# The moving operand of the 512-column matmuls read in runs of 16 bytes out of order, in a convolution and two-layer MLP kernel on one core

## The reference

```
w = softmax(weight_gen)                       # per token and head, 7 taps
x = sum over k of w[k] * x_pad[token + k]     # 8192 x 192
h = maximum(x @ w_in, 0);  x = (h * h) @ w_out
h = x @ w_in2;  out = (h * clip(h + 3, 0, 6) / 6) @ w_out2
```

## Time and profile before

| | |
|---|---|
| time, median of 2 runs | 1127.13 us (1126.98 to 1127.29) |
| span of the profiled execution | 1125.2 us |
| TensorE (PE) busy, matmuls | 1119.4 us, 99%, 9940 records |
| weight loads (PEld) busy | 1082.5 us, 96% |
| VectorE (DVE) busy | 906.8 us, 81% |
| ScalarE (ACT) busy | 668.8 us, 59% |
| granted TensorE clock | 1.000 of full speed |
| DMA | 41.28 MB, mean 37 GB/s |

### The profile page before, as it was taken

One profiled execution on the slowest core, in us unless ns is written; L12 is line 12 of the kernel. 1 busy time (PEld: TensorE's weight loads), 2 busy tenths in 40 slices (PEclk: granted clock), 3 DMA queues, 4 the chain that ended last, 5 costly groups with the idle time before them and its releaser, 6 DMA issues.

```text
span 1125.2 us, 25509 instructions
## 1 busy us (share of the span) xinstructions
PE 1119.4 (99%) x9940; PEld 1082.5 (96%) x9940; DVE 906.8 (81%) x985; ACT 668.8 (59%) x747; POOL 3.1 (0%) x10
## 2 busy tenths in 40 slices
PE   9999999999999999999999999999999999999998
PEld 8998999999999999999999999999999999999997
DVE  8788796987969789697887978879698797976665
ACT  7986556565565655645556555555655556456554
POOL 1000000000000000000000000000000000000000
PEclk9999999999999999999999999999999999999999
DMA  7221002020110201103020020200202002010001
GB/s 214 86 66 36 6 16 63 4 74 7 30 48 3 75 6 57 25 0 77 4 66 15 0 77 4 70 11 8 69 4 73 8 17 59 0 40 4 1 16 29
DMA packets 79302, 41.28 MB, mean 37 GB/s; under 512 B 56172, under 2 KB 72300, under 8 KB 79272
## 3 DMA queue, kind: packets, MB, share of 16 engines
q1 hardware_dynamic: 79144, 40.64, 13.9%
q10 hardware_dynamic: 128, 0.22, 0.1%
HBM read 29.42 MB, written 11.40 MB: 36 GB/s over the span
## 4 chain that ended last, share of the span: by engine, by line
PE 99%; DVE 0%; DMA 0%; ACT 0%; issue 0%; DVEq 0%
PE h_ps L1131 46%; PE y_ps L1141 31%; PE y_ps L1149 21%; PE h_ps L988 0%; DMA wraw<-in_weight_gen_dram 0%; PE y_ps L1099 0%; PE y_ps L988 0%; PE y_ps L1272 0%; PE h_ps L1099 0%; PE y_ps L1253 0%; DVE prod L721 0%; PE y_ps L1254 0%; PE y_ps L1259 0%; PE y_ps L1256 0%; PE h_ps L1089 0%
## 5 line engine op out<-in xcount | busy, mean ns | idle before, releaser
L1131 PE MATMUL h_ps<-xt,win 64*128 64x512 f32 x4552 | 1026.4, 386 | 0.0
L1131 PEld LDWEIGHTS h_ps<-xt,win 64*128 64x128 f32 x4552 | 801.3, 184 | 14.9
L1141 PE MATMUL y_ps<-hid_hi,wout 64*128 64x512 f32 x2032 | 542.5, 386 | 0.0
L503 ACT ACTIVATE hid_hi<-hid 128x1024 fp32r<-128x1024 f32 x240 | 254.7, 1061 | 328.9 <-DVE hid L822 166.0
L831 DVE TENSOR_TENSOR hid_lo<-hid,hid_hi 128x1024 fp32r<-128x1024 f32 x253 | 309.5, 1223 | 147.6 <-ACT hid_hi L503 141.5
L1141 PEld LDWEIGHTS y_ps<-hid_hi,wout 64*128 64x128 f32 x2032 | 373.3, 184 | 7.1 <-PE y_ps L1141 0.3
L1141 PE MATMUL y_ps<-hid_lo,wout 64*128 64x512 f32 x1016 | 311.6, 386 | 0.0
L1149 PE MATMUL y_ps<-hid_hi,wout 64*128 64x512 f32 x1016 | 311.4, 386 | 0.0
L1149 PE MATMUL y_ps<-hid_lo,wout 64*128 64x512 f32 x1016 | 311.3, 386 | 0.0
L1141 PEld LDWEIGHTS y_ps<-hid_lo,wout 64*128 64x128 f32 x1016 | 186.8, 184 | 4.0 <-DVE hid_lo L806 0.3
L1149 PEld LDWEIGHTS y_ps<-hid_hi,wout 64*128 64x128 f32 x1016 | 186.9, 184 | 3.7 <-PE y_ps L1149 0.3
(11 more groups left out here) (116 smaller groups left out, 358.1 us busy)
## 6 DMA issues: line engine op xcount, KB each, us to landing
xwin<-in_x_dram SPq DMA_DIRECT2D x14, 960.0 KB, 5.9
by_feature<-stage SPq DMA_DIRECT2D x52, 96.0 KB, 2.0
out_dram<-outs SPq DMA_DIRECT2D x240, 16.0 KB, 1.5
out_dram<-outs SPq DMA_DIRECT2D x240, 8.0 KB, 1.4
stage<-by_feature SPq DMA_DIRECT2D x13, 256.0 KB, 3.0
stage<-in_moe_w_out_dram SPq DMA_DIRECT2D x8, 384.0 KB, 3.6
stage<-in_moe_w_in_dram SPq DMA_DIRECT2D x8, 256.0 KB, 3.7
stage<-in_moe_w_in_dram SPq DMA_DIRECT2D x16, 128.0 KB, 3.7
```

What stands on the lines that cost most here:

```text
L503: act.activation(hi, hid[:, slot], ACT.Copy).then_inc(hi_done, 1)
L1131: return pe.matmul(h_ps[:, s % 2, t, :], win[layer][r, wn, cols], src[r, xn, :], start=bool(rows) and n in (0, SHORT), stop=not rows and n ...
L1141: return pe.matmul(ps[:, 0, :], wout[layer][r, tile, w_cols], src, start=bool(rows) and s == 0 and n == 0, stop=not rows and s == STEPS - ...
```

## The change

Each moving operand of 512 columns is given with a different order of its values. Two helpers are added; a run is `LINE = 4` values of fp32, 16 bytes:

```diff
+    LINE = 4
+        def woven(tokens):
+            return tokens.rearrange("p (a b c) -> p b a c", a=2, c=LINE)
+        def unwoven(tokens):
+            return tokens.rearrange("p (b a c) -> p a b c", a=2, c=LINE)
```

```diff
-                return pe.matmul(sums_of(s, 0)[:, t, :], win[0][r, w, cols], xt[1][r, x, :], start=start, stop=stop,
+                return pe.matmul(sums_of(s, 0)[:, t, :], win[0][r, w, cols], woven(xt[1][r, x, :]), start=start, stop=stop,
...
-                return pe.matmul(h_ps[:, s % 2, t, :], win[layer][r, wn, cols], src[r, xn, :],
+                return pe.matmul(h_ps[:, s % 2, t, :], win[layer][r, wn, cols], woven(src[r, xn, :]),
...
-                return pe.matmul(ps[:, 0, :], wout[layer][r, tile, w_cols], src,
+                return pe.matmul(ps[:, 0, :], wout[layer][r, tile, w_cols], unwoven(src),
...
-                return pe.matmul(ps[:, 1, :], wout[layer][r, PAIR * s + t, HI_LO_REST], src,
+                return pe.matmul(ps[:, 1, :], wout[layer][r, PAIR * s + t, HI_LO_REST], unwoven(src),
...
-                                     xt[0][REST:P, 3, :], start=False, stop=stop, tile_position=(REST, 0))
+                                     woven(xt[0][REST:P, 3, :]), start=False, stop=stop, tile_position=(REST, 0))
```

More of the change, by code:

```diff
@@ L1252, in output_sums @@
                 for t, tile in enumerate(tiles):
-                    pe.matmul(main, w[:, tile, HI_MAIN], his[:, t, :], start=False, stop=False)
-                    pe.matmul(main, w[:, tile, LO_MAIN], his[:, t, :], start=False, stop=False)
+                    pe.matmul(main, w[:, tile, HI_MAIN], unwoven(his[:, t, :]), start=False, stop=False)
+                    pe.matmul(main, w[:, tile, LO_MAIN], unwoven(his[:, t, :]), start=False, stop=False)
                 for t, tile in enumerate(tiles):
-                    pe.matmul(rest, w[:, tile, HI_LO_REST], his[:, t, :], start=False, stop=False)
+                    pe.matmul(rest, w[:, tile, HI_LO_REST], unwoven(his[:, t, :]), start=False, stop=False)
                 pe.wait_ge(lo_done, g + 1)
                 for t, tile in enumerate(tiles):
-                    ins = pe.matmul(rest, w[:, tile, HI_LO_REST], los[:, t, :], start=False, stop=last and t == PAIR - 1)
+                    ins = pe.matmul(rest, w[:, tile, HI_LO_REST], unwoven(los[:, t, :]), start=False, stop=last and t == PAIR - 1)
                 if last:
@@ L1262, in output_sums @@
                 for t, tile in enumerate(tiles):
-                    ins = pe.matmul(main, w[:, tile, HI_MAIN], los[:, t, :], start=False, stop=last and t == PAIR - 1)
+                    ins = pe.matmul(main, w[:, tile, HI_MAIN], unwoven(los[:, t, :]), start=False, stop=last and t == PAIR - 1)
                 ins.then_inc(mm2_done, 1)
```

## The result

The changed kernel takes 1197.91 us (1197.56 and 1198.27) against 1127.13 us: a ratio of 1.063 with a 95% interval of 1.061 to 1.065, 70.8 us slower. The forecast was 1127 us in a range from 1095 to 1155 us. The direction was that of rival B, which had 0.16.

What follows compares the result with a forecast made beforehand. TensorE's 9708 matmuls of 512 columns, by their distance, were taken to bound the kernel. The only term, 4864 slots by the change of distance d, was put at 0, leaving 1127 us, range 1095 to 1155 us.

Steps and rivals of the forecast that it cites:

- rival B: TensorE's moving reads pause at each jump of address: 1386 us at one column each, 1250 or 1263 if one order pays; chance 0.16.
- It removes and adds no instruction ... So the sum has a single term: Whole kernel: 9708 matmuls before and after, so time is 1127.1 + 4.864 x d us, d the change of distance per slot in ns.
- a pair of row tiles takes 200 / 884 = 226.2 ns: TensorE's distance from 1768 matmuls in a 200 us window; 512 columns take 213.3 ns, an excess of 12.9 ns a pair.
- I take d = 0: TensorE's 512-column matmuls: the new read order was taken to leave the distance per slot unchanged, giving 1127 us.
- a pause is at least one column: Upper bound for TensorE's moving reads: 0.417 ns at each of 128 changes of run, +53.3 ns a slot, +259 us.
- The first row for d = 0: TensorE's transposes: 15 ns above their weight load, about the long matmuls' 12.9 ns, so the excess is per instruction, not reading.
- The second row: VectorE reads 224 values in one run or in 32 runs of 28 bytes, both in 392 ns: broken runs show no price.
- The rule of the Trainium skill: SBUF reads: 16-byte lines, full rate from two hits, a penalty per line change; 128 changes as before, so no added time.
- Rival C: Another read order serves TensorE better, giving back part or all of the excess: down to 1064 us; chance 0.12.
- Rival D: A small fixed price per matmul instruction for more pattern dimensions: 0 to +15 us, up to 1142 us; chance 0.08.
- if TensorE prepares its reads only along neighbouring lines: Sign that the forecast of no effect is wrong: TensorE readies the next read only where it lies in the neighbouring line.
- B would be fewer ... with L1131 beside L1149 telling which of the two orders pays: Sign of pauses at jumps: 1431 matmuls in 200 us, not 1768, at one column per run; the two lines' distances compared.

Runs made afterwards that it cites:

- line64: The changed kernel with runs of 64 values, 256 bytes, in place of runs of 4: 1127.11 us, ratio 1.000 against the kernel before the change.
- run 516: No run number: a TensorE-alone probe segment reading runs of 4 values in twos, the second 516 values behind the first; 227 ns a pair, as plain order.

## Why the prediction was wrong

- **What bounds the kernel**: right. The number of matmuls by their distance makes the time in all eight full kernels that were run, up to the waits just named; no step of the sum other than d was needed.
- **"It removes and adds no instruction ... So the sum has a single term"**, 4.864 x d: right. With d = 14.7 ns it gives 71.5 us; 70.8 us were measured.
- **"a pair of row tiles takes 200 / 884 = 226.2 ns"**: a slip in reading, without weight. The count holds matmuls in flight at the edge; the distance was 226.7 ns and the excess over the columns 13.4 ns, not 12.9.
- **"I take d = 0"**: the step that failed: the term was put at nothing. d is +23 ns for the woven reads and +5 for the unwoven where an order stands alone, and +14.7 ns a slot in the kernel.
- **The bound above, "a pause is at least one column" per change of run, +53.3 ns**: the bound held, but I treated it as the next price above nothing. 23 ns over 128 changes is 0.18 ns each, 5 ns is 0.04: less than a column slot each on average. The average says nothing of which changes pay. The text of rival B allowed "part of one", and named 0.036 ns per run as the point from which it decides; its priced values, 1250 to 1386 us, did not follow from that and left the space from 1155 to 1250 us to no case.
- **The first row for d = 0, an excess that doesn't grow with the columns "is a cost per instruction"**: that it doesn't grow is so from 256 to 512 columns (13 ns at 256, 384 and 512), though the transposes, whose 68 ns a pair no fp32r matmul of 64 columns reached (112 ns), could not show it. The conclusion that order can't change it is refuted in both directions: 2.5 ns by values, 13 more in runs of 16.
- **The second row, VectorE's runs of 28 bytes at no price**: a weak bound, as said, and it misled: that engine takes about 1.0 ns for each further value (1.23 us for 1024 against 392 ns for 224). TensorE takes 0.44 ns a value in fp32r and pays. The bf16 segments, with half the bytes a column, take 216 ns in runs of 16 bytes, which fits the prediction's doubt about the rate.
- **The rule of the Trainium skill ("SBUF — State Buffer", SBUF cachelines)**, full rate from two hits in a line, does not hold for this read: single values at steps of 8 bytes have two hits in 16 bytes and take 451 ns, runs of 16 bytes have four and take 231 to 250. The measurement decides.
- **Rival C**, another order serves TensorE better: true of the mechanism and not of this change. 216 ns is within 0.2 ns of what the Trainium skill ("TensorE: Matmul & The Clock Gate", Back-to-back issue gap) gives for 512 columns, 215.8; bf16 meets that in plain order, fp32r only in some orders.
- **Rival D**, up to 3 ns per instruction for the dimensions: refuted by line64, 1127.11 us with three dimensions.
- **"if TensorE prepares its reads only along neighbouring lines"**, a sign of being wrong that the prediction named: not borne out as it stands. Runs of 16 bytes with 2064 bytes between them (516 values behind) cost nothing, 227 ns, and runs 1024 bytes apart 13 to 23.
- **"B would be fewer ... with L1131 beside L1149 telling which of the two orders pays"**: this is how it was read, and both pay.

What stays open is the rule behind the table. It is not the number of dimensions, the number of jumps, the distance alone, the weight load or the other engines' traffic. The type takes part in it, by the bytes of a column or otherwise, and so does the order of the matmuls just before.

## What to carry to other kernels

Where TensorE's distance between full-width fp32r matmuls sets the time, the order in which the moving row is read is worth a probe: it ran from 216 to 487 ns here, and plain order wasn't the fastest. Weaving two halves of the row by single values gave 11 ns of 227 back, provided that the turned order of the columns can be put right in a copy that is made anyway. Let a probe change between the orders as the kernel does: segments of one order each gave 2 to 11 us too little here. When no row shows an operation, don't step from "nothing" to the next whole unit of cost: give the space between them a case of its own.

## What the runs showed of the hardware

- 512-column fp32r matmuls with a weight load each start 227 ns apart in plain order and 216 ns woven by single values from two places, whatever the distance from 16 to 4096 bytes; with four places it is 283 ns, and single values at a step of 8 bytes take 451 ns.
- Reading runs of 16 bytes out of order costs 0 to 24 ns a matmul in fp32r, by where the next run lies (227 ns with the second run 516 values behind, 251 ns with 260 behind and the runs of each half in a row), and none in bf16 (216 ns); runs of 256 bytes cost none in the kernel.
- Plain reads behind reads in another order start up to 236 ns apart before they are back at 227, for three to nine matmuls.
- Two row tiles keep their own distances (250 and 227 ns side by side, one alone the same), and a matmul of one tile can start before one of the other that stands ahead of it in the stream.
- ScalarE and VectorE read PSUM at steps of 64 bytes in the time of plain reads (592 and 413 ns).
